# Moving a PSUM copy ahead of a rounding, and storing the last pair's softmax factors by tile

## What is computed

```
mask   = bucket(q @ proj) == bucket(k @ proj)
attn   = softmax(where(mask, q @ k.T / 8, -1e9)) @ v           (2, 8, 768, 64)
x      = attn with the heads side by side                       (1536, 512)
h      = x @ w_in1;  g = (a0 + a1 h + a2 h^2 + a3 h^3) / (1 + |b0||h| + |b1| h^2 + 1e-6);  x2 = g @ w_out1
h      = x2 @ w_in2; g = h - tanh(h);                           out = g @ w_out2
```

## Time and profile before

| what | us |
|---|---|
| median of three runs | 769.14 (769.12 to 769.36) |
| the profiled execution | 766.7 |
| its span | 764.9 |
| PE busy | 751.3 |
| DVE busy | 536.3 |
| ACT busy | 477.1 |
| POOL busy | 159.5 |

### The profile page before, as it was taken

The page is one execution under the profiler, slowest core; times in us unless marked ns, Lnnn a source line. Parts: engine busy times, 40 slices in busy tenths (PEclk is TensorE's granted clock), DMA queues, the critical chain, the costliest instruction groups (busy, mean ns, idle before and its releaser), DMA issues.

```text
span 764.9 us, 11961 instructions
## 1 busy us (share of the span) xinstructions
PE 751.3 (98%) x3840; PEld 642.4 (84%) x3840; DVE 536.3 (70%) x854; ACT 477.1 (62%) x938; POOL 159.5 (21%) x137
## 2 busy tenths in 40 slices
PE   5999999999999999999999999999999999999998
PEld 3899999999998888778888888888888888888886
DVE  4888988988997999999988898955442322233222
ACT  5989988988997888688766876755332222222221
POOL 5784665566578000000000000000000000000000
PEclk9999999999999999999999999999999999999999
DMA  8678778877645500000000133320000100001001
GB/s 196 145 172 203 172 177 186 187 177 180 159 125 162 175 1 1 0 1 1 0 1 15 55 90 103 94 86 1 0 1 1 56 0 1 0 1 56 0 1 56
DMA packets 65243, 58.11 MB, mean 76 GB/s; under 512 B 31792, under 2 KB 50480, under 8 KB 65200
## 3 DMA queue, kind: packets, MB, share of 16 engines
q1 hardware_dynamic: 63488, 57.09, 29.8%
q10 hardware_dynamic: 1712, 0.46, 0.3%
HBM read 29.57 MB, written 3.19 MB: 43 GB/s over the span
## 4 chain that ended last, share of the span: by engine, by line
PE 84%; DVE 12%; issue 2%; ACT 1%; ACTq 0%
PE acc L835 28%; PE h_ps L806 27%; PE slot L255 9%; PE turn_ps L381 8%; PE pv_ps L339 4%; PE pv_ps L341 4%; DVE pol L1000 2%; DVE sqr L979 2%; DVE pol L1011 1%; DVE pol L986 1%; DVE pol L992 1%; DVE sqr L1003 1%; PE aux_ps L268 1%; DVE g_lo L1024 1%; DVE wout_lo L1040 1%
## 5 line engine op out<-in xcount | busy, mean ns | idle before, releaser
L806 PE MATMUL h_ps<-x_hi,win_lo 128*128 128x512 f32 x384 | 149.7, 390 | 0.0
L806 PE MATMUL h_ps<-x_lo,win_hi 128*128 128x512 f32 x384 | 149.4, 389 | 0.0
L806 PE MATMUL h_ps<-x_hi,win_hi 128*128 128x512 f32 x384 | 149.4, 389 | 0.0
L856 ACT ACTIVATE g_hi<-pol 128x512 fp32r<-128x512 f32 x96 | 60.8, 634 | 125.7 <-PE acc L835 100.4
L1024 DVE TENSOR_TENSOR g_lo<-pol,g_hi 128x512 fp32r<-128x512 f32 x96 | 66.0, 687 | 97.9 <-ACT g_hi L856 97.7
L622 DVE TENSOR_TENSOR pt_lo<-turn_ps,pt_hi 128x384 fp32r<-128x384 f32 x192 | 97.9, 551 | 18.7 <-ACT pt_hi L529 17.2
L529 ACT ACTIVATE pt_hi<-turn_ps 128x384 fp32r<-128x384 f32 x192 | 84.0, 493 | 15.4 <-PE turn_ps L381 14.1
L580 DVE TENSOR_REDUCE row_min<-slot 128x1 f32<-128x768 f32 x96 | 90.5, 944 | 1.5 <-PE slot L255 1.5
L461 ACT ACTIVATE E<-slot,row_min 128x768 f32<-128x768 f32 x96 | 87.9, 915 | 4.2 <-DVE row_min L580 2.6
L806 PEld LDWEIGHTS h_ps<-x_lo,win_hi 128*128 128x128 f32 x384 | 72.1, 188 | 15.1
L806 PEld LDWEIGHTS h_ps<-x_hi,win_lo 128*128 128x128 f32 x384 | 72.1, 188 | 14.9
(11 more groups left out here) (119 smaller groups left out, 1378.6 us busy)
## 6 DMA issues: line engine op xcount, KB each, us to landing
win_raw<-in_moe_w_in SPq DMA_DIRECT2D x32, 256.0 KB, 3.5
wout_raw<-in_moe_w_out SPq DMA_DIRECT2D x32, 256.0 KB, 3.3
q_nat<-in_q SPq DMA_DIRECT2D x16, 192.0 KB, 3.2
v_nat<-in_v SPq DMA_DIRECT2D x8, 384.0 KB, 3.4
k_nat<-in_k SPq DMA_DIRECT2D x14, 192.0 KB, 3.5
qA<-q_hi SPq DMA_DIRECT2D x14, 192.0 KB, 2.5
qB<-q_hi SPq DMA_DIRECT2D x14, 192.0 KB, 2.9
qB<-q_lo SPq DMA_DIRECT2D x14, 192.0 KB, 3.2
```

The costliest lines, as they stand in the source:

```text
L806: mm = eng.matmul(h_ps[t % 4][:, :], w[:, ws], columns(x, kt, c), start=kt + n == 0, stop=kt == KT - 1 and n == 2)
L856: eng.activation(g_hi[:, t % TEMPS, :], pol[:, t % TEMPS, :], ACT.Copy).then_inc(mlp_sems["g_hi"], 1)
```

## The change

Two parts. In the first layer's steps of ScalarE, `act_x2` now stands ahead of the rounding of g. For the last pair, row_inv is written to HBM in tile order, one number at a time, and VectorE's multiplication reads the factors without steps.

```diff
@@ act_step
                 if reads:
                     act_reads(eng, t)
+                act_x2(eng, t)
                 if t >= 2:
                     act_g_hi(eng, t - 2)
-                act_x2(eng, t)
                 if t >= 1:
                     act_inverse_ln(eng, t - 1)
@@ dve_last_x
-                eng.tensor_tensor(by_tile(last_x()), by_tile(last_x()), by_tile_of_row(last_scale()),
-                                  ALU.mult).then_inc(mlp_sems["last_norm"], 1)
+                eng.tensor_tensor(last_x(), last_x(), last_scale(), ALU.mult
+                                  ).then_inc(mlp_sems["last_norm"], 1)
@@ scale_out
-                    eng.dma_start(scale_d[e].rearrange("(r t) -> r t", t=T), row_inv[:, e, :]
-                                  ).then_inc(loads[f"scale_out{e}"], 16)
+                    last = isinstance(p, int) and p == PAIRS - 1
+                    to = "(t r) -> r t" if last else "(r t) -> r t"
+                    eng.dma_start(scale_d[e].rearrange(to, t=T), row_inv[:, e, :],
+                                  allow_slow_non_contiguous=last).then_inc(loads[f"scale_out{e}"], 16)
```

## The result

The changed kernel takes 770.41 us against 767.89 us (medians of 22 runs each, taken in turn; the medians ahead of the prediction were of the first three). The ratio is 1.0033, 95% interval 1.0025 to 1.0041: slower by 2.5 us (1.9 to 3.1). The forecast was 1.65 us faster.

What follows compares the result with a forecast made beforehand. TensorE was taken as the bound, busy 751.3 of 764.9 us. Gains of 0.66 (L968), 0.97 (copies) and 0 (write) sum to 1.63 us, taken as 1.65: 769.14 to 767.5 us, range 767.2 to 768.8.

Steps and rivals of the forecast that it cites:

- What bounds the kernel: TensorE throughout; only closing its holes, or shortening VectorE work behind one, gains; from 340 us nothing can gain.
- the three later holes: TensorE's waits at 311.04, 317.08 and 339.83 us, costing 0.20, 0.60 and 0.97 us, 1.77 in sum.
- Parts 1 and 2: L968 reading its factors without steps gains 0.66 us; ScalarE's copies ahead of the rounding of g gain 0.97.
- The wait of VectorE at L1024: In step 19, VectorE would wait some 0.6 us for ScalarE's later rounding of g, at no cost.
- Part 3: The last pair's factors written by tile, 784 packets: 0.3 to 1 us longer, hidden by other waits, cost zero.
- The upper bound is the mean packet of the queue: Write by tile at 57 ns a packet: 2.8 us, 2.7 more than now, delaying weight loads by 0.3 us.
- the lower end: Write by tile at 8.5 ns a packet: 784 packets take 0.42 us, 0.3 more than now.
- Rival 3: Slow write delays weights, moving GpSimd's splits beside VectorE: slower by 0.6 us at 0.2 us a packet; chance 0.07.
- break-even: Loss from late GpSimd splits equals the 1.65 us gain at D = 5.3, a write 7.7 us longer than now.
- D: How many us late SyncE is with the weights after the first write; GpSimd's splits end that much later.
- my 0.31 us per us: VectorE's loss beside GpSimd's splits: 1.4 us lost in the 4.5 us from 242.38 to 246.91.

Runs made afterwards that it cites:

- experiment 2: Kernel before with ScalarE's new order and L968 reading without steps, factors still written by row (last pair's order wrong): 765.27 us, ratio 0.9979.
- experiment 3: Kernel before with only the write by tile added, ScalarE's order and L968 as before: 770.28 us, ratio 1.0051 to the kernel before.
- experiment 9: Changed kernel with the write's 768 packets of 4 bytes going to places 64 bytes apart in HBM: one execution, 765.75 us.

## Why the prediction was wrong

**What bounds the kernel**: right from 340 us on, where TensorE never waits. That "what is gained ahead of 340 us comes out at the end unchanged" holds only where nothing further on waits already: the 4.7 us lost at 256 us come out as 2.9, since the three later holes close behind them.

**Parts 1 and 2**: right in mechanism and size, 1.63 us forecast and 1.6 us measured together (0.6 to 2.5, experiment 2); in its trace the three holes fall from 1.77 to 0.08 us. In the changed kernel they had nothing left to gain, as experiment 3 shows. L968 fell to 0.95 us. The wait of VectorE at L1024 was 0.47 instead of 0.6 us.

**Part 3**: here it failed, at the sentence "The upper bound is the mean packet of the queue". I priced the write by the time of its packets, 0.42 to 2.8 us, and put its cost at nothing. The packets were as cheap as the lower end said (7.4 ns), and the write still landed 8.3 us later. Landing is not the last packet's end: 9.4 us lay between them. The prediction had the rows to warn of that, and I left them out: before, the 144 packets took 0.08 us of sixteen engines and the write landed after 2.5. The bound should have been on the landing, and no row of before bounds it for small crowded packets. So the range should have been open on the slow side.

The Trainium skill's rule (DMA: Bandwidth & Descriptors, Rules for kernel authors), one descriptor for each element of a strided last dimension, agrees with the 784 packets that were recorded. By its warning I would have kept away from the change. But the count is not what costs here, as experiment 9 shows with 2.6 us for the same count. The read-modify-write under 512 B (same page, Specifications) holds for the 4-byte packets of experiment 9 as well, so that rule alone does not tell the slow write from the quick one. It would fit packets that have to take turns on one stretch of HBM; no run here shows what the memory does.

**Rival 3** was this chain from the late weights on, with a chance of 0.07, though it looked for the time in the packets (0.16 us each, where they took 7.4 ns). Its break-even was just passed: it asked for a write 7.7 us longer, and it was 8.3. By its price the change would have been about even (D of 5.9 us, 1.8 lost, 1.65 gained). It lost 4.7 at TensorE instead, for three reasons. GpSimd ended 6.5 us later on the clock of the layers (255.64 less the 2.2 us of attention, against 246.9). Operations of VectorE that stand wholly beside GpSimd lose 1.0 us each, and at least three of those were among the few in front of g_lo of step 0; my 0.31 us per us was a mean over a stretch that was mostly undisturbed, and the hole grew by 3.1 us in 6.5. And the hole brought 1.65 us of half clock with it, which the prediction did not think of. The price also added the loss and the gain as if each stood alone; they do not, since the lost time closes the same three holes.

The sum as it should have stood: +3.1 for the hole at `pe_g2(0)`, +1.6 for the clock, and -1.77 for the three holes, which close whether or not parts 1 and 2 are there. That is +2.9 in the profiled execution against 2.5 (1.9 to 3.1) measured.

## What to carry to other kernels

Price a DMA that is waited for by issue to landing, not by its packets, and ask how crowded its destination in HBM is: a small write crowded into 3 KB held up SyncE and also the loads behind it, on either queue. A thing that is needed late (here at 307 us) belongs behind the loads that are needed early; moving it there turned 2.5 us of loss into 2.0 of gain. Where an engine's work moves, look at what it will then run beside: GpSimd's splits were the same work and did harm only in their new place. And holes one behind the other are not to be added: time lost at an early one gives the other engines the lead that closes the later ones.

## What the runs showed of the hardware

- 768 packets of 4 bytes into 3 KB of HBM: packets over within about 1.5 us of the issue, landed after 10.8 us. The same to places 64 bytes apart: 2.6 us (one execution).
- While such a write is outstanding, the first loads of 256 KB behind it land after 7.8 and 8.3 us on the same queue and 9.4 and 10.2 us on another, instead of 3.7 and 4.1.
- VectorE beside GpSimd: operations of 0.7 us took up to 1.76 us, GpSimd's casts of 0.61 us 1.07.
- TensorE, after holes of 3.1 to 3.5 us (five runs), started its matmuls 0.43 us apart for about 3 us, at a granted clock of 0.50 to 0.52; after a hole of 1.65 us it did not (clock 1.00).
